# The last 64 features of the first product as matmuls of 64 rows, two tiles of d_ff side by side

## The reference

```python
w = exp(weight_gen - max) / (sum + 1e-9)             # per token, head; over 7 taps
x = einsum('bshk,bskhg->bshg', w, x_unfolded)        # 16384 x 192
h = x @ w_in                                         # 192 -> 2048
g = s * maximum(h, 0.0) ** 2 + b
out = g @ w_out                                      # 2048 -> 192
```

## Time and profile before

| | us |
|---|---|
| three runs, median (lowest, highest) | 1239.95 (1239.42, 1240.96) |
| profiled execution: span from first to last instruction | 1238.8 |
| one step in the middle, transposes to transposes | 37.37 |
| PE matmul busy, share of the span | 98% |
| DVE busy, share | 78% |
| ACT busy, share | 61% |

### The profile page before, as it was taken

One profiled execution on the slowest core, in us unless ns is written; L12 is line 12 of the kernel. 1 busy time (PEld: TensorE's weight loads), 2 busy tenths in 40 slices (PEclk: granted clock), 3 DMA queues, 4 the chain that ended last, 5 costly groups with the idle time before them and its releaser, 6 DMA issues.

```text
span 1238.8 us, 18906 instructions
## 1 busy us (share of the span) xinstructions
PE 1208.1 (98%) x6880; PEld 1098.3 (89%) x6880; DVE 966.5 (78%) x1130; ACT 757.7 (61%) x812; POOL 187.3 (15%) x97
## 2 busy tenths in 40 slices
PE   3799999999999999999999999999999999999998
PEld 3699998999998999999999999999999999999998
DVE  6887778887778887778787778877778877778843
ACT  3456656656665666665665665665666665566564
POOL 7411011110011110111110111110111110111110
PEclk8899999999999999999999999999999999999999
DMA  6111101111101111101111101111101111001000
GB/s 190 36 49 35 49 16 45 48 48 35 48 13 48 48 48 35 48 13 48 48 43 41 48 13 48 48 35 48 40 21 48 48 35 48 27 34 48 13 1 26
DMA packets 17892, 51.51 MB, mean 42 GB/s; under 512 B 2140, under 2 KB 8539, under 8 KB 17882
## 3 DMA queue, kind: packets, MB, share of 16 engines
q1 hardware_dynamic: 17733, 50.80, 11.9%
q10 hardware_dynamic: 149, 0.59, 0.2%
HBM read 38.79 MB, written 12.58 MB: 41 GB/s over the span
## 4 chain that ended last, share of the span: by engine, by line
PE 96%; DVE 2%; POOL 1%; DMA 0%; issue 0%; ACTq 0%; ACT 0%; DVEq 0%; POOLq 0%
PE hp L627 47%; PE op L640 33%; PE op L642 15%; PE hp L611 1%; PE hp L614 1%; DMA x_in<-in_x 0%; POOL tap_pool L312 0%; POOL acc L321 0%; DVE x_in L187 0%; DVE g_lo L527 0%; DVE acc L498 0%; DVE acc L483 0%; DVE tap L483 0%; DVE out_sb L544 0%; DVE w_exp L451 0%
## 5 line engine op out<-in xcount | busy, mean ns | idle before, releaser
L640 PE MATMUL op<-wo,g_hi 128*128 128x384 f32 x2048 | 598.4, 362 | 7.0 <-DVE g_lo L527 7.0
L627 PE MATMUL hp<-xT,w_hi 128*128 128x512 f32 x1536 | 522.9, 395 | 1.9 <-DVE xT L511 1.9
L642 PE MATMUL op<-wo,g_lo 128*128 128x192 f32 x2048 | 514.2, 251 | 0.0
L378 ACT ACTIVATE r<-hp 128x1024 f32<-128x1024 f32 x256 | 260.4, 1017 | 360.0 <-PE hp L627 351.4
L527 DVE TENSOR_TENSOR g_lo<-r,g_hi 128x1024 fp32r<-128x1024 f32 x256 | 343.5, 1342 | 98.0 <-ACT g_hi L389 93.5
L627 PE MATMUL hp<-xT,w_lo 128*128 128x512 f32 x1024 | 402.8, 393 | 0.0
L642 PEld LDWEIGHTS op<-wo,g_lo 128*128 128x128 f32 x2048 | 393.2, 192 | 4.5
L640 PEld LDWEIGHTS op<-wo,g_hi 128*128 128x128 f32 x2048 | 385.9, 188 | 11.0 <-issue 7.4
L627 PEld LDWEIGHTS hp<-xT,w_hi 128*128 128x128 f32 x1536 | 279.5, 189 | 56.0 <-DVE xT L511 2.3
L382 ACT ACTIVATE r<-r 128x1024 f32<-128x1024 f32 x256 | 271.2, 1059 | 7.1
L627 PEld LDWEIGHTS hp<-xT,w_lo 128*128 128x128 f32 x1024 | 192.9, 188 | 42.9
(11 more groups left out here) (40 smaller groups left out, 270.8 us busy)
## 6 DMA issues: line engine op xcount, KB each, us to landing
x_in<-in_x SPq DMA_DIRECT2D x30, 960.0 KB, 4.8
out<-out_sb SPq DMA_DIRECT2D x31, 384.0 KB, 2.3
w_in<-in_weight_gen SPq DMA_DIRECT2D x32, 112.0 KB, 2.0
wo_raw<-in_moe_w_out SPq DMA_DIRECT2D x4, 384.0 KB, 7.9
w_raw<-in_moe_w_in SPq DMA_DIRECT2D x4, 256.0 KB, 6.4
w_raw<-in_moe_w_in SPq DMA_DIRECT2D x8, 128.0 KB, 6.3
x_in<-in_x SPq DMA_DIRECT2D x1, 768.0 KB, 8.1
x_in<-in_x ACTq DMA_DIRECT2D x1, 540.0 KB
```

The lines of the kernel that those rows point to most:

```text
L378: nc.scalar.activation(r[:, b, :], hp[:, PAIR * b:PAIR * (b + 1), :], ACT.Relu).then_inc(relu_done, 1)
L627: mm = nc.tensor.matmul(hp[:, j, :], w[:, f], xt, start=(n == 0), stop=(n == len(passes) - 1))
L640: nc.tensor.matmul(op[:, t, 0:2 * D], g_hi[:, g % 2, j, cols], wo[:, k, :, :].rearrange("p a d -> p (a d)"), start=(k == 0), stop=False)
L642: mm = nc.tensor.matmul(op[:, t, 0:D], g_lo[:, g % 2, j, cols], wo[:, k, 0, :], start=False, stop=(k == FT - 1))
```

## The change

The last 64 features no longer fill 128 rows with two parts. `xT2` gets two planes, the high and the low part, and each plane holds the 64 features twice: in partitions 0 to 63 and again in 64 to 127. The weights `w2_hi` and `w2_lo` are held once: even tiles of d_ff in the upper half of the partitions, odd tiles in the lower half, so they have half the columns. A pass over these features is now a matmul of 64 rows, and each tile takes three of them (hi x hi, hi x lo, lo x hi) in place of two of 128 rows. Even and odd tile alternate, in the two halves of the array and into two banks. `first_product` runs its twelve passes of 128 rows over all four tiles first, then the twelve of 64 rows.

ScalarE copies the high part to the lower partitions, behind a wait on its own earlier write; VectorE does the same for the low part; and TensorE waits for both in group 0, between its passes of 128 rows and those of 64.

```diff
@@ hi_of_attn (ACT)
                 high.then_inc(t_hi_ready, 1)
+                act.wait_ge(t_hi_ready, 2 * i + 2)
+                nc.scalar.activation(xT2[D2:P, 0, :], xT2[0:D2, 0, :].bitcast(F32), ACT.Copy).then_inc(t_hi_up_ready, 1)
@@ lo_of_attn (DVE)
                 low.then_inc(t_lo_ready, 1)
+                dve.wait_ge(t_lo_ready, 2 * i + 2)
+                nc.vector.tensor_copy(xT2[D2:P, 1, :], xT2[0:D2, 1, :].bitcast(F32)).then_inc(t_lo_up_ready, 1)
@@ load_w1 (SP); hi_of_w1 and split_w1 use half_cols in the same way
+                by_parity = moe_w_in[P:D, cols].rearrange("d (m h c) -> d m h c", h=2, c=P)
+                half_cols = slice(g * PAIR * P, (g + 1) * PAIR * P)
                 for half in range(2):
-                    sp.dma_start(w2_raw[half * D2:(half + 1) * D2, cols], moe_w_in[P:D, cols]).then_inc(w1_loaded[g], FETCH)
+                    sp.dma_start(w2_raw[half * D2:(half + 1) * D2, half_cols].rearrange("d (m c) -> d m c", c=P),
+                                 by_parity[:, :, half, :]).then_inc(w1_loaded[g], FETCH)
@@ first_product (PE)
-                    passes = [(w1_hi, xT1[:, 0, :]), (w1_hi, xT1[:, 1, :]), (w1_lo, xT1[:, 0, :]),
-                              (w2_hi, xT2[:, :]), (w2_lo, xT2[:, :])]
+                    passes = [(w1_hi, xT1[:, 0, :]), (w1_hi, xT1[:, 1, :]), (w1_lo, xT1[:, 0, :])]
                     for n, (w, xt) in enumerate(passes):
-                        mm = nc.tensor.matmul(hp[:, j, :], w[:, f], xt, start=(n == 0), stop=(n == len(passes) - 1))
-                    if j % PAIR == PAIR - 1:
-                        mm.then_inc(h_ready, 1)
+                        nc.tensor.matmul(hp[:, j, :], w[:, cols[j]], xt, start=(n == 0), stop=False)
+
+                if g == 0:
+                    pe.wait_ge(t_hi_up_ready, i + 1)
+                    pe.wait_ge(t_lo_up_ready, i + 1)
+                for m in range(PAIR):
+                    f = slice((g * PAIR + m) * P, (g * PAIR + m + 1) * P)
+                    passes = [(w2_hi, 0), (w2_hi, 1), (w2_lo, 0)]
+                    for n, (w, part) in enumerate(passes):
+                        for half in range(2):
+                            rows = slice(half * D2, (half + 1) * D2)
+                            mm = nc.tensor.matmul(hp[:, PAIR * m + half, :], w[rows, f], xT2[rows, part, :],
+                                                  start=False, stop=(n == len(passes) - 1))
+                    mm.then_inc(h_ready, 1)
```

More of the change, by code:

```diff
@@ L71, in mix_and_mlp @@
         w1_raw = sb("w1_raw", [P, F])
-        w2_raw = sb("w2_raw", [P, F])
+        w2_raw = sb("w2_raw", [P, F // 2])
         w1_hi = sb("w1_hi", [P, F], F32R)
         w1_lo = sb("w1_lo", [P, F], F32R)
-        w2_hi = sb("w2_hi", [P, F], F32R)
-        w2_lo = sb("w2_lo", [P, F], F32R)
+        w2_hi = sb("w2_hi", [P, F // 2], F32R)
+        w2_lo = sb("w2_lo", [P, F // 2], F32R)
         wo_raw = sb("wo_raw", [P, FT, D])
@@ L98, in mix_and_mlp @@
         xT1 = sb("xT1", [P, 2, N], F32R)
-        xT2 = sb("xT2", [P, N], F32R)
+        xT2 = sb("xT2", [P, 2, N], F32R)
         r = sb("r", [P, 2, PAIR * N])
@@ L149, in mix_and_mlp @@
         t_lo_ready = sem("t_lo_ready")
+        t_hi_up_ready = sem("t_hi_up_ready")
+        t_lo_up_ready = sem("t_lo_up_ready")
         h_ready = sem("h_ready")
@@ L291, in split_w1 @@
                 nc.gpsimd.tensor_tensor(w1_lo[:, cols], w1_raw[:, cols], w1_hi[:, cols].bitcast(F32), ALU.subtract)
-                nc.gpsimd.tensor_tensor(w2_lo[:, cols], w2_raw[:, cols], w2_hi[:, cols].bitcast(F32),
+                nc.gpsimd.tensor_tensor(w2_lo[:, half_cols], w2_raw[:, half_cols], w2_hi[:, half_cols].bitcast(F32),
                                         ALU.subtract).then_inc(w1_lo_ready, 1)
@@ L368, in hi_of_attn @@
                 for e in range(2):
-                    high = nc.scalar.activation(by_token(xT2[0:D2, :], e), block_b(e), ACT.Copy)
+                    high = nc.scalar.activation(by_token(xT2[0:D2, 0, :], e), block_b(e), ACT.Copy)
                 high.then_inc(t_hi_ready, 1)
+                act.wait_ge(t_hi_ready, 2 * i + 2)
+                nc.scalar.activation(xT2[D2:P, 0, :], xT2[0:D2, 0, :].bitcast(F32), ACT.Copy).then_inc(t_hi_up_ready, 1)
             def relu(i, q, first=False):
@@ L418, in hi_of_w1 @@
                 cols = slice(g * GROUP * P, (g + 1) * GROUP * P)
+                half_cols = slice(g * PAIR * P, (g + 1) * PAIR * P)
                 act.wait_ge(w1_loaded[g], 3 * FETCH)
                 nc.scalar.activation(w1_hi[:, cols], w1_raw[:, cols], ACT.Copy)
-                nc.scalar.activation(w2_hi[:, cols], w2_raw[:, cols], ACT.Copy).then_inc(w1_hi_ready, 1)
+                nc.scalar.activation(w2_hi[:, half_cols], w2_raw[:, half_cols], ACT.Copy).then_inc(w1_hi_ready, 1)
             def hi_of_wo(g):
@@ L510, in lo_of_attn @@
                 for e in range(2):
-                    low = nc.vector.tensor_tensor(by_token(xT2[D2:P, :], e), block_b(e), by_token(xT2[0:D2, :].bitcast(F32), e),
-                                                  ALU.subtract)
+                    low = nc.vector.tensor_tensor(by_token(xT2[0:D2, 1, :], e), block_b(e),
+                                                  by_token(xT2[0:D2, 0, :].bitcast(F32), e), ALU.subtract)
                 low.then_inc(t_lo_ready, 1)
+                dve.wait_ge(t_lo_ready, 2 * i + 2)
+                nc.vector.tensor_copy(xT2[D2:P, 1, :], xT2[0:D2, 1, :].bitcast(F32)).then_inc(t_lo_up_ready, 1)
             def split_g(i, q, first=False):
@@ L618, in first_product @@
             def first_product(i, g, first=False):
+                cols = [slice((g * GROUP + j) * P, (g * GROUP + j + 1) * P) for j in range(GROUP)]
                 for j in range(GROUP):
@@ L622, in first_product @@
                         pe.wait_ge(relu_done, i * PAIRS + q - 1)
-                    f = slice((g * GROUP + j) * P, (g * GROUP + j + 1) * P)
-                    passes = [(w1_hi, xT1[:, 0, :]), (w1_hi, xT1[:, 1, :]), (w1_lo, xT1[:, 0, :]),
-                              (w2_hi, xT2[:, :]), (w2_lo, xT2[:, :])]
+                    passes = [(w1_hi, xT1[:, 0, :]), (w1_hi, xT1[:, 1, :]), (w1_lo, xT1[:, 0, :])]
                     for n, (w, xt) in enumerate(passes):
-                        mm = nc.tensor.matmul(hp[:, j, :], w[:, f], xt, start=(n == 0), stop=(n == len(passes) - 1))
-                    if j % PAIR == PAIR - 1:
-                        mm.then_inc(h_ready, 1)
+                        nc.tensor.matmul(hp[:, j, :], w[:, cols[j]], xt, start=(n == 0), stop=False)
[11 more added lines that the diff above has]
+                    mm.then_inc(h_ready, 1)
             def second_product(i, g, first=False, last=False):
```

## The result

The changed kernel takes 1248.1 us (median of 4 runs, 1246.55 to 1249.54) against 1240.09 before: ratio 1.0064, 95% interval 1.0052 to 1.0076. The profiled execution has a span of 1247.7 us, 8.9 more than that of before.

The account below looks back on a forecast made before the run. TensorE was taken as the bound in steady steps. 31 boundaries at +0.27 us (+8.4) and -0.2 in the last step took the span from 1238.8 to 1247.0; with 1.2 to the median, 1248 us, range 1213 to 1303.

Parts of the forecast that it names:

- The slots: First product on TensorE: 12 full and 6 paired slots of 0.2305 us, 4.15 us in place of 4.61.
- loads whole first: Rival: weight loads must finish before their pass, so 64-row passes start 0.19 us apart; 1303 us, chance 0.06.
- not side by side: Rival: 64-row passes do not overlap, a group has 24 slots, 5.53 us; 1358 us, chance 0.07.
- The changes of tile size: TensorE switches to 64 rows and back in each group, at 0.16 us for each switch.
- the dearer sum: Whole-kernel forecast with 0.25 us for each tile-size switch: +0.88 us a step, +27.8 in all, 1268 us.
- d: End of each group's 64-row phase: second tile of the first pair runs about one load behind the first, 0.09 us.
- the case on the other side: Rival: tile-size switches free or nearly, under 0.09 us, so the kernel gets faster, about 1222 us; chance 0.32.
- The first pair and the transposes: Later first pair delays relu of pair 6 and attn_b; transposes start 5.03 us into F3, where before 4.61.
- The copies: Added ScalarE copy (at most 0.59 us) and VectorE copy (0.35), plus 0.1 wait each: hidden, not on the path.
- The low parts: Awaited by F0, done 1.0 us before it; slack shrinks to about nothing: 0 taken, up to 0.1 us a step in range.
- The start of the kernel: Start and end of the kernel left as they are, 1 us either way.

Follow-up runs that it names:

- the run on one half: Changed kernel with all 64-row passes on partitions 0 to 63, for odd tiles too, so none can overlap (wrong sums): 1403.12 us.
- the changes added pair by pair: Changed kernel with each pair of tiles running its six 128-row then six 64-row passes, four tile-size changes a group, not two: 1282.98 us.
- the order alone: Kernel of before with each group's twelve passes over xT1 first, then eight 128-row passes over xT2; no 64-row matmuls, no copies: 1257.9 us.
- half after half: Changed kernel with the even tile's three 64-row passes ahead of the odd tile's three, instead of alternating: 1249.24 us.

## Why the prediction was right, step by step

**The slots.** Right. Full passes stay at 0.23 apart, pairs of 64 rows stream at the same distance, a first product has 18 slots. The two rivals against it (loads whole first, not side by side) are out: by the timeline of the changed kernel, and by the run on one half, which is what the second of them would have cost: 1403 us. The prediction priced it at 1358, 45 too low, because it left the changes of tile size out of that sum (0.41 a group are 52 us in the whole kernel); its range of 1213 to 1303 did not hang on it.

**The changes of tile size.** The sum of a group was right, its parts were not. The prediction had 0.16 for each change and 0.09 for the second tile running behind the first, 0.41 together. The 0.16 was my estimate, a full pass's record less its slot (0.395 - 0.2305); the 0.25 of the dearer sum has the 0.09 from load to pass on top. No run shows a term of either size for a change. What the runs show is 0.2: 0.10 of gap and 0.08 to 0.11 of a load that began only with its own pass (639.68 and 639.69), and 0.20 for each of the changes added pair by pair. The two tiles start together, so d is near 0: a pair's record is 0.40 long (640.94), as a single full pass's is (639.36). 2 x 0.2 is again 0.4, and by the difference of one group's product, 4.56 - 4.15, it is 0.41. Two wrong terms made up for each other, and the case on the other side had its border at 0.11 for a change, well away.

**The first pair and the transposes.** Right, and shown by taking it apart: the order alone costs 17.7 us in the old kernel, and putting it right gains 16.4 in the new one. The transposes start 5.05 us into F3, 5.03 was said. That they agree so closely is in part luck: attn_b ended earlier than the sum had it (631.41 - 626.49 = 4.92 into F3, for 4.98), and the transposes came 0.13 after its end, where 0.05 had been put in for the semaphore; no run shows 0.05 at this place, and behind relu, in the run of the order alone, it was 633.96 - 633.85 = 0.11. The chain from relu of pair 4 to attn_b took 631.41 - 621.24 = 10.17 us, for 10.18. Left out was what each stop of TensorE costs beyond its length. In the changed kernel F0 did not stop, so the step came to 37.70 for a predicted 37.64; where it did stop, in the run of the order alone, I was 6 us too low.

**The copies.** Right: hidden. VectorE's copy began at 636.62 and was done 2.6 us before the passes that need it at 639.69. The two copies took 0.63 us on ScalarE (from 635.73) and 0.42 on VectorE, and began 0.03 and 0.04 behind the ends of the writes that they wait for (635.70 and 636.58), where the prediction had at most 0.59 and 0.35, with 0.1 for each wait. The low parts, whose slack was to go to about nothing, were done 0.2 us before F0 began at 636.81.

**The start of the kernel.** It was left as it was, and gave some back: 31 steps of 0.33 are 10.2 us, the span grew by 8.9. The 1.3 are in the first step. TensorE waited 7.0 us for the split there; now it waits 1.9 for relu and then 2.3 for the split, and its first second product starts at 44.32 instead of 45.98. Of these 1.7 us a good half is left at the next transposes (67.01 before, 66.10 now). The length of this step went with the granted clock as well: it was 0.50 from 46.00 to 51.50 before and from 44.30 to 50.70 now, but 1.00 over the same work in the profile of half after half, whose first step is 38.40 us long, where the changed kernel's is 41.36. The prediction had nothing of this, so a part of the agreement of 1248.1 with 1248 is luck: the step was 0.06 too low, 2 us in all, and the first step gave 1.3 back.

## What to carry to other kernels

Two matmuls of 64 rows in the two halves of the array cost one slot of 0.23 us here, but each change between 64 and 128 rows cost 0.2 us, near the 0.23 of a 512-column pass: count slots saved against changes made, and put many passes behind one change. When passes are put in another order for this, look at which result now comes last and who waits for it: here the order alone cost 17.7 us in the old kernel, more than the whole change did, and another order of the same matmuls turned +0.6% into -0.7%. A TensorE that was the only bound has hidden how near the other chains are; work out their arrival before you shorten it.

## What the runs showed that was not expected

- Matmuls for the idle half of the array started ahead of program order: three for one half and then three for the other ran as three pairs, 1249.2 us beside 1248.1 alternating.
- The two weight loads of a pair of halves shared one record's time, 0.19 us (640.71); they were not 0.11 apart as I had reckoned.
- A stop of TensorE cost 0.05 to 0.1 us beyond its length: 0.2 us a step in the run of the order alone, with its two stops, 0.06 in the changed kernel, with one.
- The first step of the same passes differed by 3 us between two profiles, with the granted clock at 0.50 or at 1.00 behind TensorE's waits there (41.36 and 38.40 us, the changed kernel and half after half).
